# Three stages on one core: masked heads with full-row score passes, float32 value products and an earlier hash; expert folds as transposes

## What is computed

```python
# stage 1: 16 heads (2 x 8) of width 64, attention inside hash buckets
q_bits = (q @ proj > 0); k_bits = (k @ proj > 0)        # 6 bits each
mask = bucket(q_bits)[:, None] == bucket(k_bits)[None, :]
scores = where(mask, q @ k.T / 8, -1e9)
attn = softmax(scores); x = attn @ v
# stage 2: mixing over tokens, then an MLP over 512 channels
u = x + (x.T @ U @ V).T
x = u + relu(u @ w_ch1) @ w_ch2                          # 512 -> 2048 -> 512
# stage 3: 4 experts of width 64, causal attention, top 2 of 4 gates
for e in range(4):
    y = softmax(causal(x @ wq[e] @ (x @ wk[e]).T / 8)) @ (x @ wv[e]) @ wo[e]
    out += gate[e] * y
```

## Time and profile before

| | |
|---|---|
| median of three runs | 779.01 us |
| the profiled execution | 781.1 us, its span 779.3 us |
| TensorE matmul busy | 743.0 us (95%) |
| VectorE, ScalarE, GpSimd busy | 419.9, 407.1, 204.1 us |
| mean granted TensorE clock | 0.993 of 2.4 GHz |
| stage 1 | 0 to about 318 us |
| stage 2 | about 318 to 604 us |
| stage 3 | about 604 to 779 us |

### The profile page before, as it was taken

One profiled execution on the slowest core, in us unless ns is written; L12 is line 12 of the kernel. 1 busy time (PEld: TensorE's weight loads), 2 busy tenths in 40 slices (PEclk: granted clock), 3 DMA queues, 4 the chain that ended last, 5 costly groups with the idle time before them and its releaser, 6 DMA issues. The chain is left out here.

```text
span 779.3 us, 12823 instructions
## 1 busy us (share of the span) xinstructions
PE 743.0 (95%) x4160; PEld 572.2 (73%) x4160; DVE 419.9 (54%) x938; ACT 407.1 (52%) x872; POOL 204.1 (26%) x186
## 2 busy tenths in 40 slices
PE   6999999999999999999999999999999979999986
PEld 3566666666666666688888888888888968888875
DVE  3888888888888886431112111121111667787472
ACT  2666666666666666443333333333333656677663
POOL 2322222222222230135453545444544000000000
PEclk9999999999999999999999999999999989999999
DMA  2111111111111297020000000000000000000102
GB/s 86 42 42 41 41 40 40 40 40 44 56 52 49 57 258 227 0 56 0 0 0 0 0 0 0 0 0 0 0 0 1 28 0 1 1 1 28 55 1 82
DMA packets 37788, 27.48 MB, mean 35 GB/s; under 512 B 23424, under 2 KB 31744, under 8 KB 37760
## 3 DMA queue, kind: packets, MB, share of 16 engines
q1 hardware_dynamic: 37760, 27.12, 11.9%
HBM read 23.97 MB, written 3.15 MB: 35 GB/s over the span
## 5 line engine op out<-in xcount | busy, mean ns | idle before, releaser
L860 DVE SCALAR_TENSOR_TENSOR hid_l<-psT,hid_h 128x512 fp32r<-128x512 f32 x48 | 33.2, 692 | 212.1 <-ACT hid_h L836 212.1
L405 ACT ACTIVATE pt_h<-psT 128x384 fp32r<-128x384 f32 x192 | 84.1, 489 | 92.7 <-PE psT L308 90.5
L484 DVE TENSOR_TENSOR pt_l<-psT,pt_h 128x384 fp32r<-128x384 f32 x192 | 98.8, 550 | 24.5 <-ACT pt_h L405 23.9
L413 ACT ACTIVATE probs<-psS,scale_bias 128x768 f32<-128x768 f32 x96 | 95.3, 993 | 20.4 <-DVE scale_bias L476 20.1
L466 DVE TENSOR_REDUCE negmax<-psS 128x1 f32<-128x768 f32 x96 | 91.6, 954 | 22.0 <-PE psS L295 21.4
L884 POOL TENSOR_TENSOR w_l<-w_raw,w_h 128x512 fp32r<-128x512 f32 x48 | 62.1, 1293 | 134.3 <-ACT w_h L827 134.3
L291 PE MATMUL psS<-qk_in,q 64*128 64x384 f32 x384 | 88.5, 538 | 3.5 <-ACT probs L413 3.5
L308 PEld LDWEIGHTS psT<-ident,probs 128*128 128x128 f32 x576 | 63.4, 142 | 33.0 <-DVE pt_l L484 17.5
L308 PE MATMUL psT<-ident,probs 128*128 128x128 f32 x576 | 82.9, 280 | 0.4 <-DVE pt_l L484 0.4
L827 ACT ACTIVATE w_h<-w_raw 128x512 fp32r (+1 forms) x48 | 30.3, 631 | 95.2 <-PE psS L793 95.2
L327 PE MATMUL psO<-pt_h,v_hlh 128*128 128x384 f32 x192 | 72.3, 377 | 5.4 <-DVE bits L495 5.4
(11 more groups left out here) (173 smaller groups left out, 1429.7 us busy)
## 6 DMA issues: line engine op xcount, KB each, us to landing
qk_in<-qk SPq DMA_DIRECT2D x16, 576.0 KB, 3.8
w_raw<-w SPq DMA_DIRECT2D x16, 256.0 KB, 6.5
w_raw<-w SPq DMA_DIRECT2D x4, 1024.0 KB, 8.6
raw_v<-v_n SPq DMA_DIRECT2D x16, 192.0 KB, 4.0
out<-y_out SPq DMA_DIRECT2D x12, 256.0 KB, 2.0
wvg_raw<-wv SPq DMA_DIRECT2D x4, 128.0 KB, 2.9
wqk_raw<-wq SPq DMA_DIRECT2D x4, 128.0 KB, 2.8
wqk_raw<-wk SPq DMA_DIRECT2D x4, 128.0 KB, 3.1
```

Source lines behind the costliest of these rows:

```text
L405: nc.scalar.activation(pt_h[:, TH * c:TH * (c + 1), j * P:(j + 1) * P], psT[:, c, 0:HALF].rearrange("p (t q) -> p t q", q=P), ACT.Copy).th ...
L413: nc.scalar.activation(probs[j % 2][:].rearrange("p (c n) -> p c n", c=2), psS[:, score_slot(p, j), :, 0:HALF], ACT.Exp, bias=scale_bias[: ...
L484: nc.vector.tensor_tensor(pt_l[at], psT[:, c, 0:HALF].rearrange("p (t q) -> p t q", q=P), pt_h[at].bitcast(F32), ALU.subtract).then_inc(lo ...
```

## The change

In stage 1:

- The input of a head is laid out anew: `raw` holds queries and keys on partitions 0 to 63, keys and keys on 64 to 127 (768 KB a head, before 576). One hash (`hash_both`, two full float32 products) gives the bits of queries and keys, and takes one turn of the score slots. It is issued behind the head's first score tile and one set of transposes, ahead of the previous head's first value product.
- A score tile is four fp32r products over all 128 partitions: `q_lh` x `k_hh` and `q_hb` x `k_lb`, for either half of the keys. These operands hold rests, rounded parts and bits together. ScalarE makes `round_q` and `copy_q`, GpSimd makes `scale_q`, `round_k`, `split_k`, `split_q`, `scale_key_bits`.
- The turned probabilities are kept once, in float32 (`pt`): ScalarE copies the first half of a tile, VectorE the second (`turn`). There are three `probs` buffers.
- `value_products` takes float32 values as loaded: six products of 64 columns for each half of the queries, the even key tiles into PSUM partitions 0 to 63, the odd ones into 64 to 127. `split_v` is gone.
- `fold` is three transposes; VectorE adds the halves (`add_halves`) into `o_sum`, GpSimd divides (`normalise`).
- SyncE loads head h + 2 when the operands of head h + 1 are done, and issues the mixer's and the MLP's loads behind a wait for the value products of head 13 (`pv_done`, 28).

In stage 3 `fold` is transposes too, `add_halves` is on VectorE, `normalise` on GpSimd, and the second copy of rounded and split keys is made by GpSimd (`double_keys`) instead of ScalarE and VectorE.

```diff
+                def next_loads(h, p):
+                    sp.wait_ge(kmask_ready, h + 1)
+                    sp.wait_ge(q_copied, h + 1)
...
+                    load_qk(sp, h + 2, p)
+                    if low_bound(h, 1):
+                        sp.wait_ge(pv_done, 2 * h)
+                    load_v(sp, h + 1, 1 - p)
...
+                sp.wait_ge(pv_done, 2 * (LAST - 2))
+                load_v(sp, LAST - 1, 1)
                 load_mixer(sp)
                 load_mlp_weights(sp)
...
-                        pe.wait_ge(exp_done, 6 * (h - 1) + 3)
+                def hash_both(h, p):
...
+                    pe.wait_ge(raw_in[p], half_count(h, p))
+                    if low_bound(h, 2):
+                        pe.wait_ge(exp_done, 6 * (h - 1))
...
-                        rows = slice(c * D, (c + 1) * D)
-                        last = nc.tensor.matmul(psS[0:D + NBP, bits_slot(p), c, 0:HALF], pj[rows, 0, :],
-                                                qk_in[p][rows, c * HALF:(c + 1) * HALF], start=True, stop=True)
-                    last.then_inc(q_hashed, 1)
+                        last = nc.tensor.matmul(psS[:, hash_slot(p), c, 0:HALF], pj[:],
+                                                raw[p][:, c * HALF:(c + 1) * HALF], start=True, stop=True)
+                    last.then_inc(hashed, 1)
...
-                            pe.wait_ge(exp_done, 6 * h - 1 + j)
...
+                            pe.wait_ge(exp_done, 6 * h - 1)
...
+                    elif j == 2:
+                        if below(h, LAST - 1):
+                            pe.wait_ge(q_bits_made, h + 2)
+                            pe.wait_ge(k_bits_made, h + 2)
...
-                        rows = slice(c * D, (c + 1) * D)
-                        nc.tensor.matmul(psS[:, slot, c, 0:HALF], q8[p][rows, q], qk_in[p][rows, S:S + HALF],
-                                         start=True, stop=False)
...
-                        last = nc.tensor.matmul(psS[:, slot, c, 0:HALF], q_bits[p][rows, q], k_bits[p][rows, :],
+                        k = slice(c * HALF, (c + 1) * HALF)
+                        nc.tensor.matmul(psS[:, slot, c, 0:HALF], q_lh[p][:, q], k_hh[p][:, k], start=True, stop=False)
+                        last = nc.tensor.matmul(psS[:, slot, c, 0:HALF], q_hb[p][:, q], k_lb[p][:, k],
                                                 start=False, stop=True)
...
+                    for c in range(2):
+                        if low_bound(h, 1) or j:
+                            pe.wait_ge(turned[c], 6 * h + j)
...
+                def value_products(h, p, c):
...
+                    for part in turned:
+                        pe.wait_ge(part, 6 * h + TH * (c + 1))
                     if c == 0:
-                        pe.wait_ge(exp_done, 6 * h + j + 1)
-                    if low_bound(h, 1) or j:
-                        pe.wait_ge(low_done, 12 * h + 2 * (j - 1) + c + 1)
+                        pe.wait_ge(raw_v_in[p], half_count(h, p))
+                    if low_bound(h, 1):
+                        pe.wait_ge(sum_done, 2 * h - 1 + c)
+                    q = slice(c * HALF, (c + 1) * HALF)
+                    for kt in range(QT):
+                        side = kt % 2
+                        last = nc.tensor.matmul(psO[side * D:(side + 1) * D, c, 0:HALF], raw_v[p][:, kt, :], pt[:, kt, q],
+                                                start=(kt < 2), stop=(kt >= QT - 2))
+                    last.then_inc(pv_done, 1)
...
-                        nc.tensor.matmul(psO[:, c, 0:HALF], v_hlh[p][:, kt, 0:P], pt_h[:, kt, q],
-                                         start=(kt == 0), stop=False)
-                        last = nc.tensor.matmul(psO[:, c, 0:HALF], v_hlh[p][:, kt, D:D + P], pt_l[:, kt, q],
-                                                start=False, stop=(kt == QT - 1))
...
-
...
-                        last = nc.tensor.matmul(psO[:, c, j * D:(j + 1) * D], o_t[:, c * HALF + j * P:c * HALF + (j + 1) * P],
-                                                con["fold"][:], start=True, stop=True)
...
+                        last = nc.tensor.transpose(psO[:, c, n * P:(n + 1) * P], o_t[:, j * P:(j + 1) * P], con["ident"][:])
...
+                    scores(h, p, 0)
+                    transposes(h - 1, 1 - p, 4)
+                    hash_both(h + 1, 1 - p)
+                    value_products(h - 1, 1 - p, 0)
+                    scores(h, p, 1)
+                    transposes(h - 1, 1 - p, 5)
+                    early_mix(h, (0, 1))
+                    scores(h, p, 2)
+                    fold(h - 1, 1 - p, 0)
+                    transposes(h, p, 0)
+                    scores(h, p, 3)
+                    value_products(h - 1, 1 - p, 1)
+                    early_mix(h, (2, 3))
+                    transposes(h, p, 1)
+                    scores(h, p, 4)
+                    transposes(h, p, 2)
+                    scores(h, p, 5)
+                    transposes(h, p, 3)
+                    fold(h - 1, 1 - p, 1)
+                    early_mix(h, (4, 5))
...
+                def turn(h, p, j):
+                    if not exists(h):
+                        return
+                    act.wait_ge(t_ready, 12 * h + 2 * j + 1)
+                    nc.scalar.activation(pt[:, 0:TH, j * P:(j + 1) * P], psT[:, 0, 0:HALF].rearrange("p (t q) -> p t q", q=P),
+                                         ACT.Copy).then_inc(turned[0], 1)
...
+                    nc.scalar.activation(q_hb[p][0:D, :], raw[p][0:D, 0:S], ACT.Copy, scale=SCALE).then_inc(q_rounded, 1)
...
+                    nc.scalar.activation(q_lh[p][D:P, :], raw[p][0:D, 0:S], ACT.Copy, scale=SCALE).then_inc(q_copied, 1)
...
+                def head(h, p):
+                    turn(h - 1, 1 - p, 4)
+                    exp(h, p, 0)
+                    round_q(h + 1, 1 - p)
+                    copy_output(h - 1, 1 - p, 0)
+                    turn(h - 1, 1 - p, 5)
+                    exp(h, p, 1)
+                    turn(h, p, 0)
+                    exp(h, p, 2)
+                    copy_q(h + 1, 1 - p)
+                    exp(h, p, 3)
+                    turn(h, p, 1)
+                    copy_output(h - 1, 1 - p, 1)
+                    turn(h, p, 2)
+                    exp(h, p, 4)
+                    turn(h, p, 3)
+                    exp(h, p, 5)
...
+                def turn(h, p, j):
+                    if not exists(h):
+                        return
+                    dve.wait_ge(t_ready, 12 * h + 2 * j + 2)
+                    nc.vector.tensor_copy(pt[:, TH:QT, j * P:(j + 1) * P], psT[:, 1, 0:HALF].rearrange("p (t q) -> p t q", q=P)
+                                          ).then_inc(turned[1], 1)
...
+                def add_halves(h, p, c):
...
+                    if low_bound(h, 1):
+                        dve.wait_ge(norm_done, 2 * h - 1 + c)
+                    nc.vector.tensor_reduce(o_sum[:, TH * c:TH * (c + 1), :],
+                                            psO[:, c, 0:HALF].rearrange("p (t a d) -> p t d a", a=2, d=D),
+                                            AXIS.X, ALU.add).then_inc(sum_done, 1)
...
+                def head(h, p):
+                    row_max(h, p, 0)
+                    scale_and_bias(h, p, 0)
+                    add_halves(h - 2, p, 1)
+                    turn(h - 1, 1 - p, 4)
+                    query_bits(h + 1, 1 - p)
+                    key_bits(h + 1, 1 - p)
+                    reciprocals(h - 1, 1 - p)
+                    row_max(h, p, 1)
+                    scale_and_bias(h, p, 1)
+                    turn(h - 1, 1 - p, 5)
+                    row_max(h, p, 2)
+                    scale_and_bias(h, p, 2)
+                    turn(h, p, 0)
+                    row_max(h, p, 3)
+                    scale_and_bias(h, p, 3)
+                    add_halves(h - 1, 1 - p, 0)
+                    turn(h, p, 1)
+                    row_max(h, p, 4)
+                    scale_and_bias(h, p, 4)
+                    turn(h, p, 2)
+                    row_max(h, p, 5)
+                    scale_and_bias(h, p, 5)
+                    turn(h, p, 3)
...
+                def round_k(h, p):
...
                     if low_bound(h, 2):
                         pool.wait_ge(scores_ready, 6 * (h - 1))
...
+                    nc.gpsimd.tensor_tensor(k_hh[p][:], raw[p][:, S:2 * S], con["one"][:].to_broadcast([P, S]),
...
+                    nc.gpsimd.tensor_tensor(k_lb[p][0:D, :], raw[p][0:D, S:2 * S], k_hh[p][0:D, :].bitcast(F32),
...
+                    nc.gpsimd.tensor_tensor(q_lh[p][0:D, :], q8[:], q_hb[p][0:D, :].bitcast(F32),
...
+                    nc.gpsimd.tensor_tensor(k_lb[p][D:P, :], bits[D:P, :], con["big"][D:P, :].to_broadcast([D, S]),
...
-                def split_v(h, p):
...
+                def normalise(h, p, c):
...
+                    nc.gpsimd.tensor_tensor(X[:, t, h, :], o_sum[:, t, :],
+                                            rinv[:, p, t].unsqueeze(2).to_broadcast([P, TH, D]),
```

(17 more changed lines are left out.)

451 lines of the change are left out of this document (170 added, 281 removed).

## The result

The changed kernel takes **732.28 us** (median of 4 runs, 731.05 to 733.43), the kernel before beside it 779.95 (777.14 to 781.06): ratio 0.939, 95% interval 0.936 to 0.942. The forecast was 724, the range 711 to 752. The profiled execution had 733.43 us; its span is 731.5.

The account below looks back on a forecast made before the run. Stage 1 was taken as bound by TensorE's own queue. Stage 1 at -48.6 and stage 3 at -7.5 sum to -56 us, giving a forecast of 724 us, range 711 to 752.

Parts of the forecast that it names:

- The deciding term: TensorE's value products in a masked head of stage 1: 2.0 us a half of the queries, 4.1 a head.
- the row halves: Two 64-row products in a score tile took 0.75 us, so ran together; column halves were assumed to do the same.
- 14.8 + 0.15 + 0.1 + 0.15 + 0.35: Stage 1 head: TensorE's queue of 14.8 us plus waits for fourth score tile, hash, tile 3's transposes, held addition: 15.5.
- the 0.35 for the addition: Stage 1: a GpSimd operation holds VectorE's row-sums addition to about 1 us, costing 0.35 before the fourth score tile.
- The copy of a half tile: VectorE's copy of half a transposed tile in stage 1, bounded between 0.40 and 0.47 us, taken as 0.42.
- The start: First scores 1.5 us later, head 0 some 12.2 instead of 15.8: head 1 starts 2.1 us earlier.
- near 27: Stretch from head 15's first scores to the batch-1 mixing: near 27 us, from 30.8 before.
- I cost it at nothing: Mixer loads moved on SyncE behind head 13's value products: no cost, covered by the whole of head 15.
- 1.1 a head: Stage 3: shorter folds and an earlier key split together gain 1.1 us in eight heads, less in those with outputs.
- VectorE and GpSimd didn't set the pace: Rival, chance 0.14: VectorE and GpSimd set stage 1's pace, a head 16.9 us, in all 744 us.
- The serial column halves (770, 821): Two rivals: column halves run one after the other, 770 us (0.12); each pass also waits for weights, 821 (0.05).
- no wait in stage 1: Low end of the forecast's own range: stage 1 without waits, -7 us, with stage 3 at -12, giving 711.

Follow-up runs that it names:

- e1: Changed kernel with the six value products of a half reordered, key tiles 0, 2, 4 and then 1, 3, 5: 752.22 us.
- e6: Changed kernel with VectorE's addition to the row sums and the reciprocals moved behind the third maximum: 730.88 us.
- e4: Changed kernel with SyncE issuing the eight mixer loads before its wait for head 13's value products: 729.96 us.
- e9: Changed kernel with stage 3's keys doubled by ScalarE and VectorE as before, folds kept as transposes: 739.01 us.
- e2: Changed kernel with the next head's hash issued behind the first value half instead of in front of it: 751.37 us.
- e11: Changed kernel with stage 1's value products dealt out in pairs, a fold, the sums addition and some copies moved: 750.06 us.
- e7: Changed kernel with ScalarE copying both halves of the third transposed tile and the last fold before the fourth tile's transposes: 732.17 us.

## Why the prediction was right, and where it was off

**What bounds, and the queue.** Right. TensorE's queue was counted at 14.8 us a head and is 14.9. Each term holds to 0.2, and the misses offset each other: scores 4.9 for 4.7, transposes 3.7 for 3.8, folds 0.7 for 0.8. The deciding term, value products at 2.0 a half by the row halves, measured 2.08, and e1 shows why. The rule of the Trainium skill that I set against it ("TensorE: Matmul & The Clock Gate", Part 3, the mechanism), that a weight load runs beside a matmul only if it goes to another row group, would have made a half 2.9. (That is the section's list; its text also lets a load into a background weight buffer go ahead, which would fit.) As the list has it, it does not hold here: the stretches of the changed kernel have 0.14 us of weight loads inside 0.30 us in which TensorE is never idle.

**The waits**, the step "14.8 + 0.15 + 0.1 + 0.15 + 0.35", were mis-sized: 1.0 instead of 0.75 by the middle head, where 15.5 had already dropped 0.05. The hash waits 0.28 (I had 0.1), tile 3's transposes 0.4 (0.15), the fourth score tile 0.31 (0.15 + 0.35). With 15.82 that is 0.32 a head and 4.5 us, the largest part of the error. Of the 0.35 for the addition e6 gives back 0.05, within what one profiled execution can tell: I charged the lock to a chain in which the tile's scores were not ready either. The copy of a half tile, taken at 0.42 between 0.40 and 0.47, has a duration of 0.55 and a pitch of 0.46 (167.58 to the maximum at 168.04), at the upper bound.

**The start** gave 1.55 instead of 2.1: head 0 took 26.44 - 13.49 = 12.95, not 12.2. The clock may have a part in the gain: in the kernel before the granted clock was 0.50 from 17.2 to 20.6, inside head 0, in the changed kernel 1.00 there. The prediction had not read that, and no run says what it was worth.

**The end of stage 1**, "near 27", was 29.0. Failed: "I cost it at nothing", of the loads moved on SyncE. I had asked when the data is needed, not when SyncE has finished issuing and lets the stage end. By e4 it is worth 1.2 to 2.1 us, most or all of the miss.

**Stage 3** was -6.2 for -7.5. "1.1 a head" is right in four gaps between heads of seven, and e9 shows the reason given for it, that the shorter folds alone are hidden. That the seven add up to 7.9, as forecast, is in part luck: 1.2 of it is the low clock of the kernel before, of which the prediction knew nothing; without it there are 6.7. The wait for the key split has not gone altogether, 1.2 us are left in the first gap. The end costs 1.8 instead of 0.8: the clock, 1.4 us, was not in the sum.

**Rivals.** VectorE and GpSimd didn't set the pace, though VectorE was busy for 14.0 us a head (70.69 of 80), not the 13 counted. It held TensorE up in e2, ScalarE did in e11, and the lock decided in e7, each time once a copy or a maximum came a little later than in the kernel as it is. The serial column halves (770, 821) fall with the pitch of 2.08. One bound was mis-added: "no wait in stage 1" is 14 x 0.7 = 9.8 us, not 7, so the forecast's own range began at 709, not 711.

Together, of the profiled executions: 4.5 in the waits, 2 at the end of stage 1, 0.5 at the start, 1.3 in stage 3: 8.3 of the span, 56 predicted and 47.8 seen.

## What to carry to other kernels

Count the queue of the engine that bounds from pitches in the trace; that part was good to 1%. Then, for what is moved on a DMA queue, ask when its engine has issued the last one before the next point where all engines meet, not only when the data lands. And when an order is changed on one engine, walk the queues of the engines that feed it: in e11 a copy behind the wrong exponential shows as 0.64 us of wait a head, about 10 us in all (no run put that copy right alone), and two waits side by side go only together.
